# A mixture-of-experts layer inside a fused kernel: six code widths for an expert in place of four, and the last expert inside the loop

## The chip, the cores and the metric

The kernel runs on one NeuronCore of a Trainium2 chip. The metric is the time of one execution on the device in microseconds (us), as a median over runs. Besides it there is one profiled execution, whose own time is given beside its span (first to last instruction). The engines are TensorE (PE: matmuls, and PEld: its weight loads), VectorE (DVE), ScalarE (ACT), GpSimd (POOL) and SyncE (SP), each with its own instruction stream; "q" behind an engine's name (PEq, PEldq) means its sequencer, which branches, loads registers and waits.

## What is computed

Three stages, one after the other, all in float32:

```python
x = attention(q, k, v)            # 2 x 8 heads x 576 x 64; pooled by 4, plus a band of |i - j| < 4
# mixture of experts: N = 1152 tokens, D = 512, E = 8 experts, F = 1024, capacity 288
logits = x @ w_gate
expert_idx = np.argmax(logits, axis=1)
gate_w = softmax(logits)[np.arange(N), expert_idx]
disp[e, counts[e]] = x[i]         # each token goes to its expert's next free row
h = np.maximum(np.einsum('ecd,edf->ecf', disp, w1), 0.0)
y = np.einsum('ecf,efd->ecd', h, w2)
out[i] = gate_w[i] * y[expert_idx[i], pos[i]]
# dense layer: 512 -> 2048 -> 512 with g = h * tanh(softplus(h))
h = x @ w_in
g = h * np.tanh(softplus(h))
return g @ w_out
```

How many tokens an expert gets depends on the data. For the reference's input the eight counts are 87, 156, 120, 158, 108, 191, 183 and 149.

## The kernel before

The kernel is written engine by engine: each engine's stream stands in a function of its own (lines 340 to 1345), and semaphores order them against each other. There is no scheduler; what stands in a stream runs in that order.

**Stages.** Attention and the router run until about 120 us. The tokens are scattered by expert to a table in DRAM (`xe_dram`, 288 rows for an expert). Then come the eight experts, from 127.8 to 278.9 us, and then three sweeps over the dense layer until the end.

**An expert.** SP loads its rows to `xg` (`load_x`) and its weights to the four units of `raw` (`load_unit`: two halves of w1, two of w2, 1 MB each, each loaded again as soon as TensorE has used it). TensorE transposes `xg` to PSUM (`transpose_x`), ACT copies it to `xe`. `hidden(e, half, w)` multiplies: for four output tiles m and four chunks c, `w1_tile(c, m)` is the weight of 128 columns and `xe[:, c, 0:w]`, of w columns, the operand that streams, 16 matmuls for each half. ACT applies the ReLU to `hid`. `result(e, half, w)` does the same with w2 and `hid[:, c, 0:w]`, again 16 matmuls for each half. So an expert has four groups of 16 matmuls, each of which the trace shows as 32 matmul records and 32 weight loads, since a float32 matmul takes two of each. Between the two groups of `result`, TensorE transposes the next expert's rows. ACT and DVE split the result into `x2H` and `x2L` for the dense layer.

**Widths.** An expert's token count is only known at run time. `tokens_of` loads it into a register (L311), and `by_width` (L313 to L322) picks code: it compares the count with the widths in `WIDTHS`, smallest first, and runs the body for the first that holds it. Each width is a copy of its own of the body in the instruction stream. On TensorE `by_width` stands around each of the four groups, on ACT and DVE once around an expert. With the capacity of 288 the list before is 128, 160, 192 and 288. The comparison's branch is in the trace at L318, as is the jump from the end of a body to the end of its group.

**The loop.** TensorE, ACT and SP run the first experts in a loop on the sequencer (`Fori`) and the last one as code of its own behind it, since it loads and transposes no next expert; DVE runs all eight in a loop. TensorE's loop is at L1289, with the seven experts 0 to 6; its branch back to the start has that line in the trace. Behind the loop stand L1291's unrolled expert 7 and then the dense layer (`ff1`, `ff_step`).

Of the kernel before, what the change touches and what calls it, by code (L numbers as in the profile page):

```python
# [21 lines left out]
E, FE = 8, 1024  # L22
# [32 lines left out]
M1 = FE // P  # L55
# [46 lines left out]
def build(nc, q, k, v, w_gate, w1, w2, w_in, w_out, consts, out, cap):  # L102
    tok_dram = nc.dram_tensor("token_of_slot", (N, 1), U32, kind="Internal").ap()
    CAP = cap
# [4 lines left out]
    REST = CAP - FULL  # L109


    WIDTHS = [w for w in (128, 160, 192) if w < CAP] + [CAP]

    ctx = ExitStack()
    with ctx:
# [3 lines left out]
        def sem(name):  # L119
            return ctx.enter_context(nc.semaphore(name))  # L120
# [105 lines left out]
        s_xe, s_h, s_hr = sem("xe_copied"), sem("h_psum"), sem("h_relu")  # L226
# [27 lines left out]
        def od_copies(n):  # L254

            _, b, c, hh = STEPS[n]
            first = 0 if b == 0 else NT // 2 + 1
            cols = slice(hh * 4 * D, (hh + 1) * 4 * D)
            if c == 0:
                return [(vwin[OD_ROWS:P, 2 * (first + u):2 * (first + u) + 2, cols], slice(32 * u, 32 * u + 32)) for u in range(3)]  # L260
            out_ = []
            for half in range(2):
                cols = slice(half * 4 * D, (half + 1) * 4 * D)
                out_.append((vwin[OD_ROWS:P, 2 * (first + 3):2 * (first + 3) + 2, cols], slice(BLK * half, BLK * half + 32)))
                out_.append((vwin[OD_ROWS:P, BPB - 1 + b:BPB + b, cols], slice(BLK * half + 32, BLK * half + 64)))
            return out_
# [42 lines left out]
        def tokens_of(eng, e):  # L309

            return eng.value_load(cnt_i[0:1, bass.ds(e, 1)], min_val=0, max_val=CAP)  # L311

        def by_width(eng, count, body, widths=WIDTHS):  # L313

            if len(widths) == 1:
                body(widths[0])
                return
            with eng.If(count <= widths[0]):  # L318
                body(widths[0])
            with eng.Else():  # L320
                by_width(eng, count, body, widths[1:])
# [427 lines left out]
        def _(dve):  # L749
# [17 lines left out]
            def pooled(t):  # L767


                def red(dst, src):  # L770
                    return V.tensor_reduce(dst, src.rearrange("p h (s f) -> p h s f", f=FACTOR), X, ALU.add)
                dve.wait_ge(s_qTc, t + 1)
                dve.wait_ge(s_kTc, t + 1)
                turn = (AHEAD * P - S) // FACTOR
                for _, b, r0, n in tok_pieces(t):
                    lo, s0, cnt = b * S + r0, r0 // FACTOR, n // FACTOR
                    qcol = s0 if b == 0 else SDP + (s0 - turn if s0 >= turn else SD + s0)
                    kcol = b * SD + s0
                    red(qdT[:, :, qcol:qcol + cnt], qT[:, :, lo:lo + n])
                    last = red(kdT[:, :, kcol:kcol + cnt], kT[:, :, HALO + lo:HALO + lo + n])  # L780
                last.then_inc(s_qd, 1)
# [228 lines left out]
        def _(pe):  # L1010
# [215 lines left out]
            def transpose_x(e):  # L1226

                pe.wait_ge(s_xg, 16 * len({0, CAP // P * P}) * (e + 1))
                for c in range(K1):
                    for r0 in range(0, FULL, P):  # L1230
                        last = T.transpose(ps[:, c, r0:r0 + P], xg[:, r0 // P, c * P:(c + 1) * P], ident)  # L1231
                    last.then_inc(s_xet, 1)
# [7 lines left out]
                last.then_inc(s_xt3, 1)  # L1240
                pe.wait_ge(s_x3c, e + 1)

            def expert(e, last):

                count = tokens_of(pe, e)
                for half in range(2):
                    by_width(pe, count, lambda w: hidden(e, half, w))
                for half in range(2):
                    by_width(pe, count, lambda w: result(e, half, w))
                    if half == 0 and not last:  # L1250
                        pe.wait_ge(s_hr, (e + 1) * M1)
                        transpose_x(e + 1)

            def hidden(e, half, w):

                if half == 0:
                    if w > FULL:
                        transpose_rest(e)
                    else:
                        pe.sem_inc(s_xt3, 1)  # L1260
                pe.wait_ge(s_raw[half], 16 * (e + 1))
                for m in range(half * (M1 // 2), (half + 1) * (M1 // 2)):
                    if m >= 4:
                        pe.wait_ge(s_hr, e * M1 + m - 3)
                    for c in range(K1):
                        if m == 0:
                            pe.wait_ge(s_xe, K1 * e + c + 1)
                        last = mm(ps[:, m % 4, 0:w], w1_tile(c, m), xe[:, c, 0:w], c == 0, c == K1 - 1)
                    last.then_inc(s_h, 1)

            def result(e, half, w):

                if half == 0:
                    pe.wait_ge(s_yc, (e + 1) * M2)
                for c in range(half * (M1 // 2), (half + 1) * (M1 // 2)):
                    pe.wait_ge(s_hr, e * M1 + c + 1)
                    if c % (M1 // 2) == 0:
                        pe.wait_ge(s_raw[2 + half], 16 * (e + 1))
                    for m in range(M2):
                        last = mm(ps[:, 4 + m, 0:w], w2_tile(c, m), hid[:, c, 0:w], c == 0, c == M1 - 1)  # L1280
                        if c == M1 - 1:
                            last.then_inc(s_y, 1)
                if half == 0:
                    last.then_inc(s_w2u, 1)
# [1 line left out]
            keep_warm(3, WARM_SCATTER)  # L1286
            pe.wait_ge(s_tab, 1)
            transpose_x(0)
            with pe.Fori(0, E - 1) as e:  # L1289
                expert(e, False)  # L1290
            expert(E - 1, True)  # L1291

            def ff1(sweep, quad, r):
                i = sweep * MF + quad * 4 + r
# [73 lines left out]
```

## Time and profile before

| | |
|---|---|
| median of 3 runs | 490.55 us (489.43 to 494.81) |
| profiled execution | 489.67 us |
| its span | 487.9 us |
| mean granted TensorE clock | 0.984 |
| PE busy (matmuls) | 454.2 us, 93% of the span |
| PEld busy (weight loads) | 421.1 us, 86% |
| DVE, ACT, POOL busy | 288.1, 213.1, 128.2 us |
| instruction queue q8 | 25 packets, 0.41 MB |
| instruction queue q14 | 12 packets, 0.10 MB |

A row of the page's groups or of a timeline gives line, engine and operation, what is written and what is read by the program's names, and the shape; behind a bar or in brackets stands the idle time of the engine before it with what ended it. "issue" as the releaser means that the engine waited for nothing that the profile shows. Matmuls overlap in the pipeline, so the distance from start to start, not the duration of one, is what a matmul costs in a row of them. Times are from the span's start.

### The profile page before, as it was taken

The numbers are of one execution on the slowest core, as the hardware profiler recorded it, in microseconds if no ns is written. First come the engines' busy times: TensorE is split into PE (matmuls) and PEld (weight loads), VectorE is DVE, ScalarE is ACT, GpSimd is POOL, SyncE is SP. The second block draws the span as 40 slices with busy tenths as digits, with TensorE's granted clock in tenths as the row PEclk, the third lists the DMA queues.
The fourth block names the chain that finished last, engine by engine and source line by source line (L and its number), as shares of the span: only waits on it lengthen the run. The fifth ranks groups of instructions, "written<-read, shape, count | busy, mean of one in ns | idle before, by whom it ended". The sixth has DMA issues, their size and how long they took to land.

```text
span 487.9 us, 10262 instructions
## 1 busy us (share of the span) xinstructions
PE 454.2 (93%) x3622; PEld 421.1 (86%) x3623; DVE 288.1 (59%) x678; ACT 213.1 (44%) x461; POOL 128.2 (26%) x121
## 2 busy tenths in 40 slices
PE   7779899788877999999999999999999999999993
PEld 7678788678877999999999989999999999999982
DVE  2867899597410111011111189988888888888883
ACT  2234543451231333332232466656666666655541
POOL 8242703512000000000000455623353333353202
PEclk9979999997999999999999999999999999999999
DMA  9997997202476898898676513421232212141001
GB/s 193 196 181 149 222 365 263 88 24 88 159 244 220 269 363 320 259 344 300 206 255 227 157 44 48 83 78 51 77 119 56 73 46 84 43 153 43 0 0 64
DMA packets 71861, 75.08 MB, mean 154 GB/s; under 512 B 32784, under 2 KB 47504, under 8 KB 71824
## 3 DMA queue, kind: packets, MB, share of 16 engines
q1 hardware_dynamic: 70096, 69.85, 49.5%
q0 software_dynamic: 1728, 4.72, 2.6%
q8 instruction: 25, 0.41, 0.4%
q14 instruction: 12, 0.10, 0.1%
HBM read 65.12 MB, written 9.44 MB: 153 GB/s over the span
## 4 chain that ended last, share of the span: by engine, by line
PE 75%; DVE 12%; issue 4%; SPq 2%; DMA 2%; ACT 2%; POOL 1%; POOLq 0%; DVEq 0%; ACTq 0%
PE ps L1014 72%; SPq L351 2%; DVE mx L800 1%; PE ps L1231 1%; DVE sm L810 1%; DVE pr L804 1%; POOL vwin L502 1%; DMA qk_tok<-in_k 1%; DMA xg<-x_by_expert 1%; DMA x_by_expert<-x_sb,xslot 1%; PE ps L1033 1%; DVE lgd L857 0%; PE ps L1027 0%; DVE oh L861 0%; PE ps L1087 0%
## 5 line engine op out<-in xcount | busy, mean ns | idle before, releaser
L526 POOL TENSOR_TENSOR wiL<-raw,wiH 128x512 fp32r<-128x512 f32 x48 | 62.0, 1295 | 258.8 <-ACT wiH L575 160.8
L1014 PE MATMUL ps<-xe,raw 128*128 128x128 f32 (+2 forms) x512 | 70.0, 298 | 4.4 <-issue 3.9
L1014 PE MATMUL ps<-hid,raw 128*128 128x128 f32 (+2 forms) x512 | 71.4, 297 | 2.4 <-issue 2.0
L1014 PEld LDWEIGHTS ps<-xe,raw 128*128 128x128 f32 x512 | 68.7, 191 | 5.2 <-issue 4.4
L1014 PEld LDWEIGHTS ps<-hid,raw 128*128 128x128 f32 x512 | 69.2, 191 | 3.0 <-issue 3.0
L1014 PE MATMUL ps<-x2H,wiH 128*128 128x384 f32 x192 | 64.9, 338 | 0.2 <-DVE x2L L930 0.2
L1014 PE MATMUL ps<-x2H,wiL 128*128 128x384 f32 x192 | 64.6, 336 | 0.0
L1014 PE MATMUL ps<-x2L,wiH 128*128 128x384 f32 x192 | 64.4, 336 | 0.0
L930 DVE TENSOR_TENSOR woL<-wo_in,woH 128x1024 f32 x8 | 9.8, 1225 | 83.2 <-ACT woH L575 83.2
L1014 PE MATMUL ps<-woH,gH 128*128 (+1 forms) x144 | 56.8, 394 | 2.0 <-DVE gL L930 2.0
L1014 PE MATMUL ps<-woL,gH 128*128 (+1 forms) x144 | 56.6, 393 | 0.0
L1014 PE MATMUL ps<-woH,gL 128*128 (+1 forms) x144 | 56.0, 389 | 0.0
L713 ACT ACTIVATE md<-mg 128x384 f32<-128x384 f32 x48 | 25.2, 526 | 43.9 <-DVE mg L985 43.8
L669 ACT ACTIVATE hid<-ps 128x128 f32<-128x128 f32 (+2 forms) x64 | 18.8, 300 | 54.1 <-PE ps L1014 52.0
L1014 PE MATMUL ps<-warmb 128*128 128x160 bf16 x422 | 37.3, 250 | 3.4 <-issue 2.3
L967 DVE TENSOR_SCALAR mu<-ps 128x384 f32<-128x384 f32 x48 | 26.7, 556 | 22.3 <-PE ps L1014 21.2
L930 DVE TENSOR_TENSOR x2L<-ps,x2H 128x128 f32 (+2 forms) x32 | 9.0, 320 | 50.2 <-ACT x2H L575 50.1
L1014 PEld LDWEIGHTS ps<-x2H,wiH 128*128 128x128 f32 x192 | 36.1, 188 | 2.2 <-issue 0.5
L1014 PEld LDWEIGHTS ps<-x2L,wiH 128*128 128x128 f32 x192 | 36.1, 188 | 1.7
L1014 PEld LDWEIGHTS ps<-warmb 128*128 128x128 bf16 x422 | 34.4, 106 | 3.6 <-issue 2.6
L1014 PEld LDWEIGHTS ps<-x2H,wiL 128*128 128x128 f32 x192 | 36.0, 188 | 0.0
L575 ACT ACTIVATE gH<-ps 128x384 fp32r<-128x384 f32 x48 | 23.6, 492 | 26.5 <-DVE ps L991 26.4
(128 smaller groups left out, 742.1 us busy)
## 6 DMA issues: line engine op xcount, KB each, us to landing
raw<-in_moe_w SPq DMA_DIRECT2D x32, 1024.0 KB, 6.2
raw<-in_moe_w_in SPq DMA_DIRECT2D x24, 512.0 KB
x_by_expert<-x_sb SPq DMA_DIRECT2D x1, 4608.0 KB, 15.7
xg<-x_by_expert SPq DMA_DIRECT2D x8, 512.0 KB, 3.6
wo_in<-in_moe_w_out SPq DMA_DIRECT2D x8, 512.0 KB, 7.0
v<-in_v SPq DMA_DIRECT2D x4, 576.0 KB
qk_tok<-in_q SPq DMA_DIRECT2D x8, 256.0 KB, 4.7
qk_tok<-in_k SPq DMA_DIRECT2D x8, 256.0 KB, 5.2
```

The costliest lines, as they stand in the source:

```text
L351: d = sp.dma_start(qk_tok[p0:p0 + n, slot3, i, :].rearrange("p (h d) -> p h d", h=H), src[b, :, r0:r0 + n, :].rearrange("h s d -> s h d"))
L502: nc.gpsimd.tensor_copy(dst, src).then_inc(s_odv, 1)
L526: nc.gpsimd.tensor_tensor(wiL[:, r, :, :], raw_wi_tile(r), wiH[:, r, :, :].bitcast(F32), ALU.subtract).then_inc(s_wil, 1)
L575: return nc.scalar.activation(dst, src, ACT.Copy)
L669: nc.scalar.activation(hid[:, m, 0:w], ps[:, m % 4, 0:w], ACT.Relu).then_inc(s_hr, 1)
L713: nc.scalar.activation(d, mg[:, r1, :], ACT.Ln, bias=2.0).then_inc(s_ln, 1)
L800: V.tensor_reduce(st(mx), sc, X, ALU.max).then_inc(s_mx, 1)
L804: V.tensor_tensor(pb, sc, st(mx).unsqueeze(3).to_broadcast(shape), ALU.subtract).then_inc(s_sub, 1)
L810: V.tensor_reduce(st(sm), pb, X, ALU.add).then_inc(s_sum, 1)
L930: V.tensor_tensor(dst, whole, high.bitcast(F32), ALU.subtract).then_inc(sem_, 1)
L967: V.tensor_scalar(mu[:, r, :], ps[:, 3 + r, 0:SW], MISH_CAP, None, ALU.min).then_inc(s_uc, 1)
L1014: return T.matmul(out_, a, b, start=start, stop=stop, skip_group_check=True)
```

## The change

```diff
@@ -109,7 +109,7 @@
-    WIDTHS = [w for w in (128, 160, 192) if w < CAP] + [CAP]
+    WIDTHS = [w for w in (96, 128, 160, 192, 224) if w < CAP] + [CAP]
@@ -1240,16 +1240,17 @@
-            def expert(e, last):
+            def expert(e):
 
                 count = tokens_of(pe, e)
                 for half in range(2):
                     by_width(pe, count, lambda w: hidden(e, half, w))
                 for half in range(2):
                     by_width(pe, count, lambda w: result(e, half, w))
-                    if half == 0 and not last:
-                        pe.wait_ge(s_hr, (e + 1) * M1)
-                        transpose_x(e + 1)
+                    if half == 0:
+                        with pe.If(e < E - 1):
+                            pe.wait_ge(s_hr, (e + 1) * M1)
+                            transpose_x(e + 1)
@@ -1286,9 +1287,8 @@
-            with pe.Fori(0, E - 1) as e:
-                expert(e, False)
-            expert(E - 1, True)
+            with pe.Fori(0, E) as e:
+                expert(e)
```

`WIDTHS` becomes 96, 128, 160, 192, 224 and 288 on TensorE, ACT and DVE. TensorE's loop runs all eight experts; an `If` on the loop's counter skips the transposes of a next expert in the last one. ACT and SP keep their last expert behind the loop. In the changed file all lines of TensorE's stream from L1251 on stand one lower.

Three places of TensorE's stream. The first is the start of the first group in the loop (`hidden`, half 0): rows of the difference, `-` before and `+` after; a row without a count is one matmul, `x13` is thirteen of them.

```order
 L318 COMPARE_AND_BRANCH
-L1261 ISA
-L1267 REGISTER_ALU
+L1262 ISA
+L1268 REGISTER_ALU
+L1014 MATMUL ps<-xe,raw 128x96
+L1268 REGISTER_ALU
+L1014 MATMUL ps<-xe,raw 128x96
+L1268 REGISTER_ALU
+L1014 MATMUL ps<-xe,raw 128x96
+L1268 REGISTER_ALU
+L1014 MATMUL ps<-xe,raw 128x96 x13
```

A body of 96 columns stands ahead of the one of 128, with 16 matmuls as that has, and each wider body one place later. The same comes in all four groups, and between 192 and 288 a body of 224. The second place is between the two groups of `result`.

```order
-L1251 ISA
+L1251 COMPARE_AND_BRANCH
+L1252 ISA
 L1228 ISA
 L1231 MATMUL ps<-cst,xg 128x128 x8
-L318 COMPARE_AND_BRANCH
-L1276 ISA
-L1278 REGISTER_ALU
+L1251 UNCONDITIONAL_BRANCH
+L318 COMPARE_AND_BRANCH
```

The eight transposes of the next expert now stand behind a branch of their own. The third place is the end of the loop before, where it closes and the unrolled last expert begins.

```order
-L1289 REGISTER_ALU
-L1289 COMPARE_AND_BRANCH
-L311 TENSOR_LOAD cnt_i
-L311 ISA x2
-L318 COMPARE_AND_BRANCH
-L1014 MATMUL ps<-xe,raw 128x128 x16
-L318 UNCONDITIONAL_BRANCH
-L318 COMPARE_AND_BRANCH
-L1014 MATMUL ps<-xe,raw 128x160 x16
```

These rows and the rest of the unrolled expert, 256 matmuls in 16 bodies, are gone; behind the closing branch, now L1290, comes the dense layer. TensorE's stream has 2,146 matmuls in its code before and 2,014 after. In the loop there are 16 bodies of 16 matmuls before and 24 after.

## Rows read from the trace of the kernel before

**Rows 1.** The page: the chain that ended last, by line.

```profile
PE ps L1014 72%; SPq L351 2%; DVE mx L800 1%; PE ps L1231 1%; DVE sm L810 1%; DVE pr L804 1%; POOL vwin L502 1%; DMA qk_tok<-in_k 1%; DMA xg<-x_by_expert 1%; DMA x_by_expert<-x_sb,xslot 1%; PE ps L1033 1%; DVE lgd L857 0%; PE ps L1027 0%; DVE oh L861 0%; PE ps L1087 0%
```

**Rows 2.** Busy time by stretch: experts 0, 1 and 5; then clock, DMA.

```profile
127.70:149.30 21.60, 15.96 (x136) 15.39 (x136) 2.23 (x5) 5.50 (x18) 0.00 (x0) 1.00 0.53 177
149.30:167.70 18.40, 18.37 (x137) 18.37 (x138) 1.31 (x2) 5.05 (x15) 0.00 (x0) 1.00 0.82 289
...
216.90:238.60 21.70, 21.69 (x136) 21.67 (x137) 2.00 (x5) 5.59 (x16) 0.00 (x0) 1.00 0.74 252
```

**Rows 3.** Timeline of PE, expert 0 and start of 1: start, us, what, [idle before].

```profile
127.80 7.41 PE L1014 MATMUL ps<-xe,raw 128*128 128x128 f32 x64 [0.55 <-ACT xe L575]
135.04 3.18 PE L1014 MATMUL ps<-hid,raw 128*128 128x128 f32 x27
138.58 0.82 PE L1014 MATMUL ps<-hid,raw 128*128 128x128 f32 x5 [0.36 <-issue]
139.24 1.04 PE L1231 MATMUL ps<-cst,xg 128*128 128x128 f32 x8
140.11 0.72 PE L1014 MATMUL ps<-hid,raw 128*128 128x128 f32 x5
142.43 3.28 PE L1014 MATMUL ps<-hid,raw 128*128 128x128 f32 x27 [1.60 <-issue]
149.33 8.96 PE L1014 MATMUL ps<-xe,raw 128*128 128x160 f32 x64 [3.62 <-issue]
```

**Rows 4.** Until 127 us: instruction packets; busy PE, PEld and the others.

```profile
q8 instruction: 12, 0.20, 0.7%
...
0.00:127.00 127.00, 108.72 (x1534) 96.56 (x1535) 96.62 (x299) 46.60 (x79) 47.91 (x55) 0.95 0.74 178
```

**Rows 5.** DMA queues, 127 to 150 us: packets, MB, share.

```profile
q8 instruction: 5, 0.08, 1.4%
```

**Rows 6.** DMA queues, 150 to 262 us; q8 has no row there.

```profile
q1 hardware_dynamic: 16224, 31.85, 82.4%
q14 instruction: 1, 0.01, 0.0%
```

**Rows 7.** DMA queues, 262 to 281 us.

```profile
q8 instruction: 4, 0.07, 1.4%
```

**Rows 8.** Branches by line (ns min/median/max, start us): 143:144; 150:262; L1289; 266:270.

```profile
L318 PEldq COMPARE_BRANCH  x1: 3706/3706/3706, 143.6 to 143.6; - x1
...
L318 PEldq COMPARE_BRANCH  x72: 64/169/213, 151.4 to 258.9; - x72
...
L1289 PEldq COMPARE_BRANCH  x7: 76/208/242, 147.4 to 257.8; - x7
...
L318 PEldq COMPARE_BRANCH  x3: 64/213/2497, 266.6 to 269.5; - x3
```

**Rows 9.** Timeline of PE, from the later experts.

```profile
158.13 4.51 PE L1014 MATMUL ps<-hid,raw 128*128 128x160 f32 x32
...
167.70 7.31 PE L1014 MATMUL ps<-xe,raw 128*128 128x128 f32 x64
174.84 3.74 PE L1014 MATMUL ps<-hid,raw 128*128 128x128 f32 x32
...
216.91 10.66 PE L1014 MATMUL ps<-xe,raw 128*128 128x192 f32 x64 [0.23 <-issue]
227.41 5.36 PE L1014 MATMUL ps<-hid,raw 128*128 128x192 f32 x32
...
260.36 8.86 PE L1014 MATMUL ps<-xe,raw 128*128 128x160 f32 x64
269.69 8.93 PE L1014 MATMUL ps<-hid,raw 128*128 128x160 f32 x64 [0.47 <-ACT hid L669]
```

**Rows 10.** The logits' matmuls, by tile, 74 to 75.1 us: ns, start.

```profile
L1014 PEld LDWEIGHTS ps<-wg,xT x8: 190/192/192, 74.1 to 74.9; 128*128 128x128 f32 x8
L1014 PE MATMUL ps<-wg,xT x8: 228/256/256, 74.2 to 75.0; 128*128 128x8 f32 x8
```

## Prediction

> **What bounds the kernel now.** I read first the chain of waits, then the busy time by stretch, then the order of time on TensorE, and last the instruction queues and the sequencer's branches. The chain says that matmuls of line 1014 end last for 72% of the span [rows 1]. In the expert stretch, 127.7 to 278.8 us, TensorE is busy without a break in experts 1 to 6: 18.4 us of 18.4 in expert 1, 21.7 of 21.7 in expert 5, at a granted clock of 1.00 [rows 2]. Only expert 0 is loose: 21.6 us with 16.0 busy. So whatever stops TensorE there is paid in full, and faster copies or loads buy nothing.
>
> The stops of expert 0 have no releaser, "issue" [rows 3]. Where they fall tells what they are. The first is after record 27 of 32 in the third group of blocks, the second after record 5 of the fourth. By the program's order, between these two points lie 5 + 5 records of two instructions each, three skipped blocks of about 71, eight transposes of two, and some ten waits and branches: about 256 instructions. The instruction queue moves pages of 16 KB, 12 of them by 127 us [rows 4], while TensorE runs 1,534 matmul records and as many weight loads [rows 4]: also about 256 instructions a page. So the stops are page borders at which the next page isn't there yet. Before 150 us five pages come [rows 5]; from 150 to 262 us none [rows 6]; then four, when the unrolled last expert and the code behind it begin [rows 7]. The loop's code is thus held while it runs. A fp32 block of 16 matmuls is 64 instructions and 6 or so others; four groups of four widths make 1,173, and the border found above puts the loop's start about 124 instructions into a page. The loop then touches 6 pages, 17 instructions of the last. With the page ahead of it, which is fetched too (five came: four of the loop's six and one more), 7 pages are held at once.
>
> What a missing page costs: the branch at 143.6 us, to the loop's last page, takes 3,706 ns where others take 169 [rows 8]; it ends at 147.27, and the first matmul of expert 1 starts at 149.33 [rows 3]. So the sequencer's way back through the loop is 2.06 us. In later turns TensorE's queue hides it: behind a 128-wide block 0.23 us shows [rows 9], behind wider ones nothing. A 128-wide record takes (174.84 - 167.70)/64 = 0.112 us, one of 160 (158.13 - 149.33)/64 = 0.1375, one of 192 (227.41 - 216.91)/64 = 0.164 [rows 3, 9]. The cover is 2.06 - 0.23, about 1.9 us or 17 records, at 128; so 2.3 us at 160 and 2.8 at 192.
>
> **The change part by part.** *The new widths.* The trace's experts run 128, 160, 128, 160, 128, 192, 192, 160 wide. The reference's input has 87, 156, 120, 158, 108, 191, 183, 149 tokens, so only expert 0 changes, to 96; 224 is never taken. What does a 96-wide fp32 record cost? The trace has none. From above: 0.112, as at 128. From below: the logits multiply 8 columns with 128-column fp32 weights, and eight such records start from 74.1 to 74.9 us (weights) [rows 10], again 0.11 each, though hardly anything streams. The weight load sets the pace there, and expert 0's weights are the same size. So 96 wide gains 0. The streaming slope, (0.1375 - 0.112)/32 columns, would give 0.085 and 128 x 0.026 = 3.4 us; the 8-column row speaks against it, and I keep it for the range.
>
> The Trainium skill's page "TensorE: Matmul & The Clock Gate" (section "LDWEIGHTS (loading the stationary operand)") says that a load takes its column count over 1.2: 107 ns for 128 columns, and the trace agrees with 0.11. The same page's section "Back-to-back issue gap" has an isolated gap that follows the moving columns alone; by that the 3.4 us would come.
>
> *One more branch.* Each chosen width of 128 and up stands one block later, in four groups and on each engine. A taken hop is about 0.27 us (208 ns [rows 8] and the compare behind it). Inside an expert the queue hides it; after a 128-wide block it shows: twice, 0.5 us.
>
> *The last expert inside.* It removes the unrolled blocks and their page stop: a branch of 2,497 ns at 266.6 us [rows 8], of which TensorE sees 269.69 - 260.36 - 64 x 0.1375 = 0.5 [rows 9]: -0.5 us. The added If costs a compare beside the transposes, hidden.
>
> *The loop's length.* Six widths instead of four: 24 blocks and the rest are 1,747 instructions. From 124 into a page that is 1,871/256 = 7.3, so 8 pages, the last one entered for the closing branch; with the page ahead 9. The trace shows 7 held, and never 8 or 9.
>
> Expert 0 meets its pages for the first time. Its block is now the first of six, so each jump to the next group passes 355 instructions, more than a page, and in groups one and four lands where nothing was fetched ahead. Group one is issued by 129.5 us; a missing page, 3.7, gives 133.2; the next about 4.4 (steps seen: 142.43 - 138.58 = 3.85, 147.27 - 142.43 = 4.84) gives 137.6; two steps of 3.85, 145.3; transposes and group four are issued by 148.1; a missing page again, 151.8; the way back 2.06, 153.9. Before: 149.33. So +4.5 us.
>
> If the ninth page drives out the loop's first, each turn of the loop meets a missing page at its jump back: 3.5 us over a usual branch, plus about 1.0 for the page ahead that is fetched first: 4.5 (bounds: 3.5, if the page ahead doesn't stand in the way, and 7.2, if the two go one after the other). First turn: 4.5. The six others, way + 0.27 + 4.5 - cover - the idle time already there: 160 to 128 wide 1.8 + 0.27 + 4.5 - 2.3 = 4.2, twice; 128 to 160 and 128 to 192 4.8 each; 192 to 192 4.3; 192 to 160 4.0. Together 26.3.
>
> Sum: 4.5 + 4.5 + 26.3 - 0.5 = 34.8 us, with the extra hops in it. The profiled execution took 489.67 us (span 487.9), within 1 us of the median 490.55, so 489.67 + 34.8 is 524 us.
>
> The Trainium skill's page "Runtime: NRT & Kernel Launch" (section "Instruction fetch mechanics") gives TensorE 128 KiB of instruction memory in blocks of 16 KiB, 8 pages: by that 9 don't fit. It also says that a taken branch out of a window of two pages always waits for its page; by that each jump back of 1,170 instructions would wait already, and the 208 ns of [rows 8] and the absent pages of [rows 6] are against it.
>
> ACT's loop grows too, from 178 to 262 instructions of its own smaller pages. It is busy 5 to 6 us of an expert [rows 2], so a late page there has room: 0.
>
> **The rivals.** *Nothing is driven out* (9 pages fit, or the page ahead isn't fetched for a stay of two instructions; against the latter: in the kernel before, the last page was left after as few, and a fifth page came [rows 5]). Then 4.5 + 0.5 - 0.5 = +4.5, 494 us.
> *Everything is driven out.* If the oldest page goes, 9 pages cycling through fewer places miss at every border. A turn of 8 pages is then seven steps of at least 3.85, a miss and the way: about 33 us instead of 18.5. Seven turns: (231 - 129.5), and 7 for the first: about 595 us, between 570 and 625. For it: expert 0 shows that chain page by page. Against: it needs replacement by age, which no row shows.
> *Faster.* One mechanism: pages for expert 0 come before they are needed, as the twelve before 127 us do [rows 4]. Then its stops, 0.36 + 1.60 + 3.62 = 5.6 us, go, and 96 wide records at 0.085 give 3.4: 5.6 + 3.4 + 0.5 - 0.5 = 9.0, 481 us. It decides from the point where a page step is shorter than a block's 3.6 us.
>
> **How the numbers follow.** That 9 pages don't all stay I take at 0.69: more than 7 are never held. One page driven out 0.45, 524 us, own range 517 (3.5 per turn) to 543 (7.2 per turn). Nothing driven out 0.26, 494. Everything 0.24, 595. Faster 0.05, 481. The range leaves out the faster case and the upper half of the 595 case: 493 to 600, 0.83. One per cent, 4.9 us, is about what a measurement of this kernel can tell. The 494 case lies at 0.9%, so two thirds of it, 0.18, is "same" and the rest slower: 0.77 slower, 0.05 faster.
>
> **What would show it.** Between 150 and 262 us, where the queue of instruction pages is empty now, two pages per turn (next page and loop start) and a branch of line 1290 of 4 to 5 us instead of 0.2; matmuls of expert 0 with 96 columns 0.112 us apart; no idle time inside experts 1 to 7. Pages at every border and stops inside the blocks would mean the 595 case; no page after the first turn the 494 case. I am wrong altogether if experts 1 to 7 run unbroken and expert 0 gets shorter than 21.6 us, or if the weights don't bind at 96.

## The result

| | before | after |
|---|---|---|
| median | 491.35 us (489.43 to 494.81, 4 runs) | 630.72 us (623.36 to 634.04, 4 runs) |
| ratio of the times | | 1.272, 95% interval 1.264 to 1.281 |
| profiled execution / span | 489.67 / 487.9 us | 627.74 / 625.9 us |
| mean granted clock | 0.984 | 0.895 |
| first expert matmul to first dense-layer matmul | 127.80 to 278.87: 151.1 us | 125.95 to 416.91: 291.0 us |
| from there to the end of the span | 209.0 us | 209.0 us |
| packets of instruction queue q8 | 25 | 86 |

The kernel became 27% slower. The ratio is of the runs without two slow ones (634.04 and 633.69 us after, more than 1.5% above the fastest), so it is a little under the ratio of the two medians. The prediction was 524 us with a range of 493 to 600, so it is wrong: the direction was right, the size was not. Behind the experts nothing changed, and before them 1.9 us; the difference, 139.9 us, lies in their stretch. The chain by engine of the kernel before, then that of the changed kernel and its queue of instruction pages:

```profile
PE 75%; DVE 12%; issue 4%; SPq 2%; DMA 2%; ACT 2%; POOL 1%; POOLq 0%; DVEq 0%; ACTq 0%
...
PE 66%; issue 18%; DVE 9%; DMA 2%; ACT 2%; POOL 1%; SPq 1%; POOLq 0%; DVEq 0%; ACTq 0%
...
q8 instruction: 86, 1.41, 1.0%
```

"issue" is now 18% of the chain, where it was 4%. The busy time of the stretch of all experts, in order PE, PEld, DVE, ACT, POOL, then clock, DMA share and GB/s; first of the kernel before:

```profile
127.80:278.87 151.07, 144.55 (x1081) 143.17 (x1081) 18.18 (x38) 46.05 (x137) 5.12 (x4) 1.00 0.75 258
```

and of the changed kernel, the whole stretch, and experts 0, 1, 5 and 7 of it, which answer to [rows 2]:

```profile
125.95:416.91 290.96, 187.36 (x1081) 181.49 (x1081) 18.32 (x38) 46.00 (x137) 5.58 (x4) 0.79 0.42 139
...
125.95:161.00 35.05, 19.32 (x137) 18.69 (x137) 2.19 (x5) 5.19 (x18) 0.00 (x0) 0.79 0.34 111
161.00:194.80 33.80, 23.37 (x137) 22.66 (x137) 2.38 (x5) 5.72 (x17) 0.00 (x0) 0.80 0.49 162
308.80:350.00 41.20, 27.57 (x136) 26.73 (x136) 2.57 (x5) 6.11 (x17) 0.00 (x0) 0.83 0.41 132
389.00:416.90 27.90, 22.79 (x128) 22.10 (x129) 1.69 (x3) 6.47 (x17) 5.58 (x4) 0.83 0.43 136
```

The number of matmul records is the same, 1,081. TensorE's idle time grew from 6.5 to 103.6 us (+97.1) and its busy time from 144.6 to 187.4 us (+42.8). The granted clock fell from 1.00 to 0.79: that is 1.2 GHz for about four tenths of the time, in many short stretches, and 2.4 GHz for the rest. Expert 1 takes 33.8 us where it took 18.4 [rows 2].

Where the idle time lies, in order of time on TensorE, against [rows 3] and [rows 9]:

```profile
125.95 3.81 PE L1014 MATMUL ps<-xe,raw 128*128 128x96 f32 x32 [0.54 <-ACT xe L575]
131.96 5.43 PE L1014 MATMUL ps<-xe,raw 128*128 128x96 f32 x32 [2.20 <-issue]
...
145.77 5.34 PE L1014 MATMUL ps<-hid,raw 128*128 128x96 f32 x32
161.00 11.60 PE L1014 MATMUL ps<-xe,raw 128*128 128x160 f32 x64 [9.89 <-issue]
176.19 6.28 PE L1014 MATMUL ps<-hid,raw 128*128 128x160 f32 x32 [3.60 <-issue]
...
183.54 4.61 PE L1014 MATMUL ps<-hid,raw 128*128 128x160 f32 x32 [0.19 <-issue]
194.79 6.57 PE L1014 MATMUL ps<-xe,raw 128*128 128x128 f32 x32 [6.65 <-issue]
205.33 6.42 PE L1014 MATMUL ps<-xe,raw 128*128 128x128 f32 x32 [3.97 <-issue]
```

At each turn of the loop TensorE stands for 6.7 to 10.4 us, and again once or more inside an expert, for up to 4.4 us. Behind the stops many records run at a lower granted clock: 32 records of 128 columns take 6.42 us at 205.33, at a granted clock of 0.58 over them, where 3.74 us did [rows 9].

What the sequencer does there. The changed kernel's queue of instruction pages in one turn, from 161.0 to 194.8 us, where the kernel before has no such row [rows 6]:

```profile
q8 instruction: 9, 0.15, 1.9%
```

and its branches: the one that closes the loop over the whole span, the width branches of one turn, and those of the first (ns min/median/max, first and last start):

```profile
L1290 PEldq COMPARE_BRANCH  x8: 76/4603/5024, 152.2 to 415.2; - x8
...
L318 PEldq COMPARE_BRANCH  x15: 69/234/3902, 164.9 to 194.3; - x15
...
L318 PEldq COMPARE_BRANCH  x3: 89/1897/3870, 127.6 to 134.8; - x3
```

Nine pages are fetched in the turn, as many as the loop's eight and the one ahead. The closing branch takes 4.6 us instead of 0.21 [rows 8], and others of this turn up to 3.9 us. The first jump of expert 0 over more than a page, at 127.6 us, takes 3,870 ns; the sum had 3.7 us for it.

### The profile page after: what moved, and what is told of

Same layout as the page of the kernel before. It is cut to its first block, busy times and chain, and to the rows that moved or that the text cites. A ratio compares the mean times of both kernels' runs of the same rounds, so it can differ in the third digit from the quotient of the medians.

```text
span 625.9 us, 10332 instructions
## 1 busy us (share of the span) xinstructions
PE 496.2 (79%) x3622; PEld 458.8 (73%) x3623; DVE 287.5 (46%) x678; ACT 212.9 (34%) x461; POOL 128.6 (21%) x121
## 4 chain that ended last, share of the span: by engine, by line
PE 66%; issue 18%; DVE 9%; DMA 2%; ACT 2%; POOL 1%; SPq 1%; POOLq 0%; DVEq 0%; ACTq 0%
PE ps L1014 64%; PE ps L1231 1%; DVE mx L800 1%; DVE sm L810 1%; DVE pr L804 1%; POOL vwin L502 1%; SPq L351 1%; DMA qk_tok<-in_k 1%; DMA xg<-x_by_expert 1%; DMA x_by_expert<-x_sb,xslot 0%; ACT hid L669 0%; PE ps L1033 0%; DVE lgd L857 0%; DVE x_sb L889 0%; PE ps L1027 0%
## 5 line engine op out<-in xcount | busy, mean ns | idle before, releaser
L1014 PE MATMUL ps<-xe,raw 128*128 128x160 f32 (+3 forms) x512 | 101.1, 376 | 76.5 <-issue 76.0
L1014 PEld LDWEIGHTS ps<-xe,raw 128*128 128x128 f32 x512 | 98.1, 259 | 79.5 <-issue 78.7
L1014 PE MATMUL ps<-hid,raw 128*128 128x160 f32 (+3 forms) x512 | 80.7, 321 | 22.4 <-issue 21.7
L1014 PEld LDWEIGHTS ps<-hid,raw 128*128 128x128 f32 x512 | 77.4, 210 | 24.9 <-issue 24.9
L669 ACT ACTIVATE hid<-ps 128x160 f32<-128x160 f32 (+3 forms) x64 | 19.0, 297 | 157.7 <-PE ps L1014 157.7
L930 DVE TENSOR_TENSOR x2L<-ps,x2H 128x160 f32 (+3 forms) x32 | 9.2, 316 | 90.3 <-ACT x2H L575 90.2
```

The lines of the kernel that those rows point to most:

```text
L669: nc.scalar.activation(hid[:, m, 0:w], ps[:, m % 4, 0:w], ACT.Relu).then_inc(s_hr, 1)
L930: V.tensor_tensor(dst, whole, high.bitcast(F32), ALU.subtract).then_inc(sem_, 1)
L1014: return T.matmul(out_, a, b, start=start, stop=stop, skip_group_check=True)
```

## The experiments

The theory from here on, P: TensorE's sequencer holds 8 pages of 256 instructions, fetches the page behind the one that it enters, and when a page comes the oldest goes. Runs that only repeat one loop can't tell whether the oldest is the one that came first or the one used last the longest ago, and nothing below needs that. A loop that touches 9 then meets each of them missing in every turn. Rivals: the added widths or their branches (W), the last expert and its If inside the loop (I), the length of the loop whatever the borders (L or S).

**One part alone: the widths (e1).** The last expert stays unrolled.

```diff
-    WIDTHS = [w for w in (128, 160, 192) if w < CAP] + [CAP]
+    WIDTHS = [w for w in (96, 128, 160, 192, 224) if w < CAP] + [CAP]
```

> The kernel before with the six widths alone; the last expert stays unrolled behind the loop. Theory P (the loop's code outgrows the pages that are held): the loop is 1,745 instructions from 124 into a page, 8 pages and the one ahead, as in the changed kernel; so about 615 to 635 us, with about 9 instruction pages fetched in each turn of the loop (six turns after the first), and the unrolled expert 7 at nearly full speed, so somewhat under the changed kernel's 631. Rival I (the last expert and its If inside the loop do it): 485 to 500 us.

Measured: 614.55 us (612.06 to 619.92, 4 runs) against 488.83 of the kernel before beside it, ratio 1.262 (1.251 to 1.273). The loop's branch, now for seven experts:

```profile
L1289 PEldq COMPARE_BRANCH  x7: 76/4842/4960, 149.7 to 375.2; - x7
```

The widths alone carry the loss, a little smaller, with six turns back to the loop's start instead of seven; the time is 0.5 us under the expected 615 to 635. One part of what was expected failed: the unrolled expert 7 doesn't run at nearly full speed. It takes 26.2 us (376.93 to 403.15) where it took 18.5, since it now meets its own pages for the first time.

**The other part alone: the last expert in the loop (e2),** with the widths 128, 160, 192 and 288.

```diff
-    WIDTHS = [w for w in (96, 128, 160, 192, 224) if w < CAP] + [CAP]
+    WIDTHS = [w for w in (128, 160, 192) if w < CAP] + [CAP]
```

> The changed kernel with the four widths of before: only the last expert runs inside the loop. Theory P: 1,175 instructions from 124 into a page are 6 pages and the one ahead, 7 as before; no page is fetched in the loop after the first turn, and the stop of 0.5 us at the unrolled expert's third group is gone: 489 to 491.5 us, not to be told from before. Rival I (the If, or the loop closing into the dense layer, stops the sequencer in each turn): over 500 us.

Measured: 488.92 us (484.25 to 492.19, 10 runs) against 488.83, ratio 1.000 (0.996 to 1.005). The branch that closes the loop takes its usual time, and no page of q8 comes in the loop after the first turn:

```profile
L1290 PEldq COMPARE_BRANCH  x8: 76/209/246, 144.2 to 274.0; - x8
```

So rival I is out. The last expert does lose its stop: it takes 17.8 us (258.73 to 276.52) where it took 18.5 [rows 9]. But behind the stop ahead of expert 1, 3.19 us here, the first 64 records take 10.50 us instead of 8.96, as the granted clock is at 1.2 GHz for part of them, and the stretch of the experts is 151.3 us long, against 151.1.

**One width less: 224, which no expert takes (e3).** What is run is the same as in the changed kernel.

```diff
-    WIDTHS = [w for w in (96, 128, 160, 192, 224) if w < CAP] + [CAP]
+    WIDTHS = [w for w in (96, 128, 160, 192) if w < CAP] + [CAP]
```

> The changed kernel without the width of 224, which no expert takes: 96, 128, 160, 192 and 288. The work done is the same, instruction by instruction. Theory P: 1,461 instructions from 124 into a page are 7 pages and the one ahead, 8; if 8 are held, no page is fetched after the first turn and the time is 491 to 497 us (the first expert is slower by the jumps over more than a page); if only 7 are held, about 600 us. Rival W (the 96-wide body or the longer chain of compares costs the time): 600 us or more, as both are still there. 96-wide fp32 matmul records stand 0.112 us apart if the weight load binds, 0.085 if the columns do.

Measured: 496.35 us (495.81 to 497.46, 4 runs) against 488.83, ratio 1.017 (1.011 to 1.023).

```profile
L1290 PEldq COMPARE_BRANCH  x8: 76/208/246, 153.1 to 284.1; - x8
```

Of a loss of 27%, 1.7% is left, and what went is code that never runs. The rest, 7.5 us, is the first expert (27.5 us instead of 21.5) and the start of the second: the timeline begins

```profile
127.73 4.48 PE L1014 MATMUL ps<-xe,raw 128*128 128x96 f32 x38 [0.57 <-ACT xe L575]
133.35 3.14 PE L1014 MATMUL ps<-xe,raw 128*128 128x96 f32 x26 [1.14 <-issue]
139.29 6.88 PE L1014 MATMUL ps<-hid,raw 128*128 128x96 f32 x32 [2.81 <-issue]
...
155.26 10.98 PE L1014 MATMUL ps<-xe,raw 128*128 128x160 f32 x64 [4.67 <-issue]
```

It meets its pages for the first time and stops for them, and after two of the stops part of the records run at half clock: 6.88 us for 32 records of 96 columns, at a granted clock of 0.52, and 10.98 us for 64 of 160, at 0.81.

**Only the borders moved (e4).** The changed kernel whole, with a piece ahead of the loop that is jumped over.

```diff
             pe.wait_ge(s_tab, 1)
+            first = tokens_of(pe, 0)
+            with pe.If(first > CAP - 1):
+                keep_warm(3, 74)
             transpose_x(0)
```

> The changed kernel whole, with 148 instructions that are jumped over put ahead of the loop (74 warm-up matmuls behind a branch that is never taken), so that the loop of 1,747 instructions begins 19 instead of 124 into a page. Theory P: it then lies in 7 pages, with the one ahead 8, as with five widths: 491 to 498 us if 8 pages are held. Rival L (it is the length of the loop in instructions, or the number of bodies, not where the page borders fall): 620 to 635 us, as before the shift.

Measured: 488.37 us (485.42 to 496.62, 10 runs) against 488.83, ratio 0.999 (0.996 to 1.003). The loop of 1,747 instructions, the six widths and the If are all there, and the time is that of the kernel before, even a little under the expected 491 to 498. Its loop branch, and the start of its expert 0:

```profile
L1293 PEldq COMPARE_BRANCH  x8: 76/208/237, 146.9 to 276.3; - x8
...
125.76 7.38 PE L1014 MATMUL ps<-xe,raw 128*128 128x96 f32 x64 [0.36 <-ACT xe L575]
136.96 7.04 PE L1014 MATMUL ps<-hid,raw 128*128 128x96 f32 x32 [3.83 <-issue]
```

The 64 records of 96 columns take 7.38 us, at a granted clock of 1.00, where 64 of 128 columns took 7.31 [rows 9]. The narrower body gains nothing; that the weight loads set the pace fits this and the 8-column row [rows 10].

**The border to within 44 instructions (e5).** The same with 96 warm-up matmuls in the skipped piece instead of 74.

```diff
-                keep_warm(3, 74)
+                keep_warm(3, 96)
```

> The shifted kernel (e4_shift) with 22 more warm-up matmuls in the part that is jumped over, 44 instructions: the loop of 1,747 now begins 63 instead of 19 into a page and ends 18 instructions into an eighth page. Theory P (9 pages cycle through 8 places, the oldest goes): 615 to 635 us again, 9 pages in each turn of the loop. Rival L (some other effect of the placing, such as how near the blocks' starts are to borders): a change of a few us, below 500.

Measured: 624.01 us (621.4 to 626.62, 2 runs) against 490.91, ratio 1.271 (1.262 to 1.280).

```profile
L1293 PEldq COMPARE_BRANCH  x8: 79/4910/5118, 157.5 to 415.5; - x8
```

Forty-four instructions that never run, outside the loop, take the ratio from 0.999 to 1.271. By the theory's count of instructions, this puts the limit between a loop that ends in its seventh page and one that ends 18 instructions into its eighth: with the page ahead, 8 pages are held and 9 are not.

**The same length in one piece (e6) or in four (e8).** Two kernels with four widths and all experts in the loop. The first has 588 skipped instructions in one place of the loop:

```diff
                 for half in range(2):
                     by_width(pe, count, lambda w: hidden(e, half, w))
+                with pe.If(count > CAP - 1):
+                    keep_warm(3, 294)
```

> The kernel with four widths and all experts in the loop (e2), and in the middle of the loop, after the second group, 588 instructions that are always jumped over (294 warm-up matmuls behind a branch never taken): the loop is 1,765 long and ends in its eighth page, but one page within the skipped piece is neither entered nor next to one that is. Theory P, counted by pages fetched: 8 in a turn, all held, 488 to 500 us. Rival S (what counts is the stretch from the loop's start to its end): over 590 us, like the changed kernel.

Measured: 491.95 us (489.49 to 495.64, 8 runs) against 490.91, ratio 1.003 (0.999 to 1.007). The second has 576 of them, in four places:

```diff
                 for half in range(2):
                     by_width(pe, count, lambda w: hidden(e, half, w))
+                    with pe.If(count > CAP - 1):
+                        keep_warm(3, 72)
                 for half in range(2):
                     by_width(pe, count, lambda w: result(e, half, w))
+                    with pe.If(count > CAP - 1):
+                        keep_warm(3, 72)
                     if half == 0:
                         ...
```

> As e6, but the skipped instructions stand in four pieces of 144, one after each group: the loop is 1,759 long, and every page of it is entered; with the one ahead 9. No width of 96 or 224 is in it, and no matmul more is run than in the kernel before. Theory P: 9 pages in each turn, over 590 us. Rival W (96 and 224 themselves, or their branches): 488 to 500 us.

Measured: 632.69 us (629.53 to 635.86, 2 runs) against 490.91, ratio 1.289 (1.279 to 1.298). The loop branch and the queue of instruction pages over the whole run, of the first and then of the second:

```profile
L1292 PEldq COMPARE_BRANCH  x8: 76/209/227, 149.9 to 278.1; - x8
...
q8 instruction: 22, 0.36, 0.4%
```

```profile
L1294 PEldq COMPARE_BRANCH  x8: 76/4680/4978, 155.0 to 417.2; - x8
...
q8 instruction: 86, 1.41, 1.1%
```

Both loops are within 6 instructions of the same length, 1,765 and 1,759, and the faster one is the longer. What differs is that a page inside the one long piece is never entered, nor is the one just before it in the code: 8 pages in a turn against 9. The queue shows it: in the first turn, from 128 us to the closing branch, 7 pages come in the second kernel and 6 by 280 us in the first, and none of these after 155 us. So it is pages fetched that count, not the stretch from start to end, and neither 96 nor 224 is needed for the loss: the second has none of them and is as slow as the changed kernel.

**A version a little faster than both (e7).** Four widths, all experts in the loop, and the skipped piece of e4 ahead of the loop.

> The kernel with four widths and all experts in the loop (e2), shifted by 152 instructions that are jumped over ahead of it, so that the loop of 1,175 begins 19 into a page and lies in 5 pages instead of 6. Theory P: the first turn doesn't wait for a sixth page at its closing branch, where the kernel before has a branch of 3.7 us and TensorE stands for 3.6: 2 to 3.5 us less than before, 485.5 to 487. If the page borders that it now meets cost the first turn as much elsewhere: no difference.

Measured: 483.91 us (483.04 to 488.46, 6 runs) against 490.91, ratio 0.986 (0.982 to 0.990): 7 us or 1.4% less, small, but clear of the interval. The expected gain was 2 to 3.5 us. In the profiled executions the stretch of the experts is 145.6 us, 5.5 shorter:

```profile
132.10:277.66 145.56, 144.00 (x1080) 143.02 (x1081) 18.17 (x38) 46.16 (x137) 5.62 (x4) 1.00 0.78 267
...
132.10 7.41 PE L1014 MATMUL ps<-xe,raw 128*128 128x128 f32 x64 [0.35 <-ACT xe L575]
139.34 3.74 PE L1014 MATMUL ps<-hid,raw 128*128 128x128 f32 x32
143.42 1.09 PE L1231 MATMUL ps<-cst,xg 128*128 128x128 f32 x8 [0.34 <-issue]
144.35 3.74 PE L1014 MATMUL ps<-hid,raw 128*128 128x128 f32 x32
148.83 8.96 PE L1014 MATMUL ps<-xe,raw 128*128 128x160 f32 x64 [0.75 <-issue]
```

The first expert stops for 0.34 and 0.75 us where it stopped for 0.36, 1.60 and 3.62 [rows 3]. I had counted only the last of the three as avoidable; most of it is gone and the second with it, 4.5 us together. The last expert's stop is gone as in e2. The profiled execution is the slowest of the six, 488.46 us, only 1.2 less than the one before, since its experts begin at 132.10 us instead of 127.80; the ten profiles of this case have them begin anywhere from 123.3 to 132.1. So the trace places 5.5 us of the gain, and the rest of the medians' difference isn't placed.

## Why the prediction was wrong, point by point

**What bounds the kernel** was right: what stops TensorE in the expert loop is paid in full. The reading of the stops as page borders, 256 instructions a page, the loop's start 124 into one, 6 pages before and 8 after, and one more ahead, is borne out by e4 and e5, the loop's start to within 44 instructions.

**"The new widths: 96 wide gains 0"** was right: 7.38 against 7.31 us for 64 records. The 3.4 us kept against it follow from the streaming slope of the prediction's own rows. By the isolated gap on the Trainium skill's page "TensorE: Matmul & The Clock Gate" (section "Back-to-back issue gap"), 1/2.4 ns for a column, they would be an estimated 1.7 us. The records show neither. **The added hops and the If** were costed at 0.5 us and can't be seen; e4 has them all at a ratio of 0.999. **The last expert inside, -0.5 us,** was about right: 17.8 us instead of 18.5 in e2's trace, and nothing that the medians can tell.

**Expert 0, +4.5 us.** The mechanism held. Its branch over a page took 3.87 us for 3.7. In e3 and e4, where no page is lost, the whole stretch of the experts is 158.9 and 153.0 us against 151.1, so +7.8 and +1.9. The size hangs on where the borders fall, and on the clock. In the changed kernel the first turn takes 35.05 us (125.95 to 161.00) where it took 21.53, +13.5; the sum had 4.5 + 4.5 = 9.0 for it.

**The step that failed** is "if the ninth page drives out the loop's first, each turn of the loop meets a missing page at its jump back": one miss a turn, 26.3 us for the six turns behind the first, given 0.45 and the forecast itself. That there would be 9 pages, more than are held, was right. But it is not one page that goes, it is each in turn: nine come in the turn from 161.0 to 194.8 us, and in e8, which shares only the page count, the time is the same (632.7 against 630.7 us). From expert 1 to the end of the experts it is 255.9 us instead of 129.5, so +126.4 where the sum had 26.3 - 0.5; with the first turn's +13.5 that is the whole 139.9. The rival "everything driven out" was the right one, and I gave it 0.24, with the words that it "needs replacement by age, which no row shows". No row showed replacement by place either. With nothing in the trace for either, the two should have stood even, and a middle forecast between 494 and 595 was a choice for the gentler mechanism, not a reading. That more than 7 pages are never held, also a premise of the sum, was wrong as well: e3, e4 and e6 hold 8.

**The term that was missing in that rival** is the clock. Its price was 33 us for a turn, from steps of 3.85, which makes (231 - 129.5) + 7 = 108.5 us and 598 us; the prediction wrote 595. All of that is idle time, and TensorE's idle time grew by 97.1 us, near it. Besides, the busy time grew by 42.8 us at the same number of records, with the granted clock at 0.79 over the stretch; 97.1 and 42.8 are the 139.9 that was measured. The prediction has no term for the clock. [rows 2] shows it at 1.00 behind a stop of 3.62 us, but that row shows one stop, and one stop can be enough: behind 3.83 us in e4 32 records run at a granted clock of 0.50, and e2 has it behind 3.19 us. In the changed kernel stops of 6.7 to 10.4 us return in each turn. How much of the 42.8 us would come back if the clock held stays open: at full clock the blocks would end sooner and TensorE might wait longer for the same pages. No run tells this apart.

**The range** of 493 to 600 left out the upper half of the right case, whose own range of 570 to 625 was itself too low, by 3 us at the profiled execution (627.74) and 6 at the median. The missing clock term is more than enough for that.

Of what the Trainium skill states, "Runtime: NRT & Kernel Launch" (section "Instruction fetch mechanics") has TensorE's instruction memory at 128 KiB in blocks of 16 KiB; the runs agree, 8 pages held and 9 not. Its rule in the same section, that a taken branch whose target is outside the current window of two pages waits for a fetch, is contradicted: in e4 the loop branch goes back from the seventh of its pages to the first in 208 ns.

## What to carry to other kernels

Code that never runs isn't free when it stands in a loop: count the loop's instructions on an engine (only TensorE was measured here), lay them on the page borders, add the page ahead, and compare with what the engine holds; if it is one page too many, expect every page to be fetched anew in every turn. A row of the instruction queue inside a loop's later turns, or a loop branch of microseconds, is the sign, and moving the loop's start by some instructions, or putting skipped code in one piece, can be the whole cure. Before adding a narrower variant of a body, look for a row in which the other operand already sets the pace.

## What the runs showed of the hardware that was not expected

- TensorE's sequencer held 8 pages of 16 KB and fetched every one anew in each turn when a loop touched 9: 86 packets of q8 in the changed kernel instead of 25, nine in a turn, and 126 to 142 us of time (e1, e5, e8 and the changed kernel stand at 614.6, 624.0, 632.7 and 630.7 us; e2, e3, e4 and e6 at 488.9, 496.4, 488.4 and 492.0).
- The branch to a missing page took 3.7 us (kernel before, 143.6 us) and 3.87 us (changed kernel, 127.6 us), and 4.5 to 5.0 us at the jump back of the changed kernel, where the page ahead is fetched as well. Other branches in its loop took up to 6.7 us (198.0 us); what they wait for besides the page no run takes apart. A full turn of nine pages took 33.8 us at the least (expert 1) and 42.3 us at the most.
- A page that the sequencer jumps past, with the one just before it in the code not entered either, is not fetched: with 588 skipped instructions in the loop 6 pages come in the first turn (e6), with 576 in four pieces 7 (e8), and the former can't be told from the kernel before (492.0 against 490.9 us, ratio 0.999 to 1.007).
- Behind stops of some microseconds TensorE's granted clock fell to 1.2 GHz: +97.1 us idle and +42.8 us busy for the same 1,081 records in the changed kernel. A single stop was enough in e2 (3.19 us) and e4 (3.83 us), but not in the kernel before (3.62 us), so the length of the last stop doesn't decide alone.
